# Output products of four of six token tiles in seven block products instead of eight

## The reference

```
kv  = einsum('bhsd,bhse->bhde', k, v)            # 4 batches, 8 heads, 576 positions, head size 64
out = einsum('bhsd,bhde->bhse', q, kv)
x   = out / sqrt(mean(out*out, -1) + 1e-6) * g_norm   # as 2304 tokens x 512
x   = (x @ w_a * (x @ w_b)) @ w_out              # layer 1: 512 -> 1536 -> 512
x   = (sigmoid(x @ w_gate) * (x @ w_val)) @ w_out2    # layer 2: the same sizes
```

## Time and profile before

| | |
|---|---|
| median of 3 runs | 926.57 us (923.29 to 927.03) |
| profiled execution, its own time | 924.99 us |
| its span, first to last instruction | 923.2 us |
| PE busy | 908.6 us, 98% |
| DVE busy | 542.2 us, 59% |
| ACT busy | 460.4 us, 50% |
| mean granted TensorE clock | 0.996 |

### The profile page before, as it was taken

How to read it: one execution, slowest core, us unless ns; L and a number is a source line. 1 busy time by engine, 2 the same in 40 slices (tenths; PEclk the granted TensorE clock), 3 DMA queues, 4 the chain that set the end, 5 groups by cost and what they waited for, 6 DMA issues and landing times.

```text
span 923.2 us, 14827 instructions
## 1 busy us (share of the span) xinstructions
PE 908.6 (98%) x5313; PEld 872.3 (94%) x5313; DVE 542.2 (59%) x1020; ACT 460.4 (50%) x943; POOL 17.5 (2%) x81
## 2 busy tenths in 40 slices
PE   8989999999999999999999999999999999999997
PEld 7979999999999999999999999988999988999986
DVE  1687987773555563555573778763556563555541
ACT  3677645453534453444453664563554553554531
POOL 1121000000000000000000000000000000000000
PEclk9998999999999999999999999999999999999999
DMA  9992365586534456544455464689554558453435
GB/s 236 246 238 80 120 229 211 192 291 213 206 137 178 164 184 227 198 146 154 165 174 180 160 215 161 208 305 310 180 184 138 195 175 299 178 180 139 158 129 189
DMA packets 85544, 177.13 MB, mean 192 GB/s; under 512 B 6368, under 2 KB 52448, under 8 KB 85472
## 3 DMA queue, kind: packets, MB, share of 16 engines
q1 hardware_dynamic: 85472, 176.19, 57.0%
HBM read 146.28 MB, written 29.88 MB: 191 GB/s over the span
## 4 chain that ended last, share of the span: by engine, by line
PE 91%; DVE 3%; DMA 2%; ACT 1%; issue 1%; POOL 0%; SPq 0%; POOLq 0%; DVEq 0%; ACTq 0%
PE bank L590 57%; PE bank L624 16%; PE bank L626 16%; DMA w_raw<-in_moe_w_a_dram 1%; PE bank L504 1%; DMA kv_in<-in_v_dram 1%; PE bank L520 1%; DVE sum_sq L885 1%; ACT squares L692 0%; DVE w_lo L965 0%; ACT x_hi L752 0%; PE bank L491 0%; DVE x_lo L970 0%; DVE t_raw L959 0%; ACT w_hi L738 0%
## 5 line engine op out<-in xcount | busy, mean ns | idle before, releaser
L590 PE MATMUL bank<-x_hi,w_hi 128*128 128x384 f32 x1008 | 342.6, 340 | 1.7 <-ACT kv L686 1.7
L590 PE MATMUL bank<-x_hi,w_lo 128*128 128x384 f32 x1008 | 342.4, 340 | 0.0
L590 PE MATMUL bank<-x_lo,w_hi 128*128 128x384 f32 x1008 | 341.3, 339 | 0.0
L590 PEld LDWEIGHTS bank<-x_hi,w_hi 128*128 128x128 f32 x1008 | 189.9, 188 | 7.5 <-issue 2.0
L590 PEld LDWEIGHTS bank<-x_lo,w_hi 128*128 128x128 f32 x1008 | 190.0, 188 | 6.8
L590 PEld LDWEIGHTS bank<-x_hi,w_lo 128*128 128x128 f32 x1008 | 190.0, 188 | 0.0
L624 PE MATMUL bank<-h_hi,wo 128*128 128x384 f32 x576 | 156.1, 335 | 0.4
L965 DVE TENSOR_TENSOR w_lo<-s_raw,w_hi 128x512 fp32r<-128x512 f32 x144 | 99.1, 688 | 78.9 <-ACT w_hi L738 78.7
L626 PE MATMUL bank<-wo,h_hi 128*128 128x512 f32 x432 | 139.2, 392 | 0.9 <-DVE wo L979 0.5
L965 DVE TENSOR_TENSOR w_lo<-w_raw,w_hi 128x512 fp32r<-128x512 f32 (+1 forms) x144 | 79.8, 554 | 88.9 <-ACT w_hi L738 88.8
L772 ACT ACTIVATE h_hi<-h 128x384 fp32r<-128x384 f32 x144 | 74.0, 521 | 81.3 <-PE bank L626 23.9
(11 more groups left out here) (63 smaller groups left out, 727.4 us busy)
## 6 DMA issues: line engine op xcount, KB each, us to landing
wo<-wo_dram SPq DMA_DIRECT2D x120, 512.0 KB, 5.0
s_raw<-s_dram SPq DMA_DIRECT2D x48, 512.0 KB, 4.5
s_dram<-s_raw SPq DMA_DIRECT2D x24, 512.0 KB, 5.3
wo_dram<-wo SPq DMA_DIRECT2D x24, 512.0 KB, 5.3
w_raw<-in_moe_w_a_dram SPq DMA_DIRECT2D x18, 512.0 KB, 3.5
w_raw<-in_moe_w_b_dram SPq DMA_DIRECT2D x18, 512.0 KB, 3.8
w_raw<-in_moe_w_gate_dram SPq DMA_DIRECT2D x18, 512.0 KB, 3.8
w_raw<-in_moe_w_val_dram SPq DMA_DIRECT2D x18, 512.0 KB, 3.5
```

The source lines that it names most:

```text
L590: last = pe.matmul(to[:, 0:HT], w[:, u % 2, at, c, :], xx[:, i, c, :], start=(OPENS[i] and c == 0 and n_pass == 0), stop=(c == 1 and n_pas ...
```

## The change

Tiles 1, 2, 4 and 5 ("fast" tiles) do `h @ w_out` with seven block products for eight. The tokens are cut in two halves, the features of h in two halves of six chunks (`FC`), and the 512 output columns in two halves of 256 (`DH_OUT`). `output_product(tau, i)`, i = 0 to 6, runs behind all 12 units; no unit of a fast tile has matmuls of the output product between its own. Tiles 0 and 3 keep `project`.

- A product is six steps; a fast tile has 42 steps for 24, each with its own `h_hi` and `h_lo`. In the first layer a step is two blocks of three matmuls of 384 columns, in the second three blocks of three matmuls of 256 columns.
- The four sums of h are made by VectorE in place (`sum_h`: 24 additions of 128x384 a tile), in the buffers of h and, for two of the four blocks, in x, whose tile is no longer read by then. The ring of `h_hi` and `h_lo` has 7 slots in fast tiles.
- The four sums of w_out are made once a layer in six jobs: in tile 0 or 3 behind v = 3, 5, 7 and 9, in tile 1 or 4 at v = 1 and 4. A job (`sum_wo`) is four additions of 128x256 on VectorE, in the following unit (`split_wo_sums`) one copy of 128x1024 on ScalarE and two subtractions of 128x512 on VectorE, and 256 KB x 2 of loads and a spill of 1 MB on SP's queue.
- The additions for the next tile's token sums (`sum_tokens`) move from v = 3, 5, 7, 9 to v = 8, 9, 10, 11, and one of them is made in place in x.
- c12 and c22 of a unit are added in place; the buffers `s5`, `u2` and `c_b` are gone.
- Behind the products stand, as in a unit, a seed (`out_seed`), two kept banks (`out_keep`), and two copies and two sums into the output (`out_drain` on ScalarE, `out_sum` on VectorE). The last tile's stores of the first token half wait for the seventh product.
- w_out is loaded 512 KB at a time, now one load for two steps in a fast tile: 21 loads for a fast tile instead of 24.

```diff
-    STEPS_OF_TILE = 2 * CHUNKS
+    FC = CHUNKS // 2
+    DIRECT_STEPS = 2 * CHUNKS
+    FAST_STEPS = 7 * FC
+    H_RING, H_RING_DIRECT = 7, 4
+    DH_OUT = D // 2
...
         c_a = sb("c_a", [P, 4, HT])
-        c_b = sb("c_b", [P, 2, HT])
...
+        wo = sb("wo", [P, WO_RING, 2, 2, DH_OUT], F32R)
+        h_parts = sb("h_parts", [P, H_RING, 2, HT], F32R)
+        h_hi, h_lo = h_parts[:, :, 0, :], h_parts[:, :, 1, :]
...
+        OUT_BANKS = ((6, 7), (2, 3), (4, 5))
...
+        SUMS_AT = ({3: 0, 5: 1, 7: 2, 9: 3}, {1: 4, 4: 5}, {})
...
+            def output_product(tau, i):
+
+                f, role = fast_index(tau), ROLE[i]
+                blocks = 2 if tau < TILES else 3
+                for c in range(FC):
+                    q = i * FC + c
+                    slot = wo_slot(tau, q // 2)
+                    if q % 2 == 0:
+                        pe.wait_ge(wo_loaded[slot], 16 * wo_loads(tau, q // 2))
+                    pe.wait_ge(h_lo_ready, step(tau, q) + 1)
+                    for a in range(blocks):
+                        k, to = out_part(tau, role, a)
+                        if c == 0:
+                            if i == 0:
+                                pe.wait_ge(act_drained, act_before(tau, 0))
+                                pe.wait_ge(dve_drained, dve_before(tau, 0))
+                            elif i == 1:
+
+                                pe.wait_ge(c12_ready, unit(tau, UNITS))
+                                pe.wait_ge(h21_ready, pair(tau, PAIRS))
+                            elif i == 2:
+                                pe.wait_ge(out_seed_ready, 2 * f + k + 1)
+                            elif i == 4:
+                                pe.wait_ge(out_u2_ready, 2 * f + k + 1)
+                            elif i == 5:
+                                pe.wait_ge(out_s5_ready, 2 * f + k + 1)
+                            elif i == 6:
+                                pe.wait_ge(dve_drained, dve_before(tau, 0) + k + 1)
+                        at = slice(a * P, (a + 1) * P)
+                        for n_pass, (hh, part) in enumerate(((h_hi, 0), (h_hi, 1), (h_lo, 0))):
+
+                            opens = OPENS[i] and c == 0 and n_pass == 0 and (tau < TILES or a != 1)
+                            flags = dict(start=opens, stop=(c == FC - 1 and n_pass == 2), skip_group_check=True)
+                            if tau < TILES:
+                                last = pe.matmul(to, wo[:, slot, q % 2, part, at], hh[:, h_slot(tau, q), :], **flags)
+                            else:
+                                last = pe.matmul(to, hh[:, h_slot(tau, q), at], wo[:, slot, q % 2, part, :], **flags)
+                        if c == FC - 1 and (a == blocks - 1 or a == blocks - 2):
+                            last.then_inc(acc_done, 1)
+                        elif c < FC - 1 and a == blocks - 1:
+                            last.then_inc(project_done, 1)
...
-                    behind = project(tau, v - lag) if v >= lag else iter(())
+                    behind = project(tau, v - lag) if v >= lag and not fast(tau) else iter(())
...
-                for q in range(CHUNKS - lag, STEPS_OF_TILE):
-                    for _ in project(tau, q):
-                        pass
+                if fast(tau):
+                    for i in range(7):
+                        output_product(tau, i)
+                else:
+                    for q in range(CHUNKS - lag, DIRECT_STEPS):
+                        for _ in project(tau, q):
+                            pass
...
+            def sum_h(tau, i, c):
+
+                if i == 1:
+                    dve.wait_ge(h12_ready, pair(tau, c) + 1)
+                    dve.wait_ge(h_lo_ready, step(tau, c) + 1)
+                    dve.tensor_tensor(h11_home(c), h12_home(tau, c), h11_home(c), ALU.subtract).then_inc(t1_ready, 1)
+                elif i == 3:
+                    dve.wait_ge(h22_ready, pair(tau, c) + 1)
+                    dve.wait_ge(t1_ready, fast_pair(tau, c) + 1)
+                    dve.tensor_tensor(h12_home(tau, c), h22_home(tau, c), h12_home(tau, c), ALU.subtract).then_inc(t3_ready, 1)
+                elif i == 2:
+                    dve.wait_ge(h_lo_ready, step(tau, FC + c) + 1)
+                    dve.tensor_tensor(h11_home(c), h22_home(tau, c), h11_home(c), ALU.subtract).then_inc(t2_ready, 1)
+                else:
+                    dve.wait_ge(h_lo_ready, step(tau, 2 * FC + c) + 1)
+                    dve.wait_ge(h21_ready, pair(tau, c) + 1)
+                    dve.tensor_tensor(h11_home(c), h21_home(c), h11_home(c), ALU.subtract).then_inc(t4_ready, 1)
+
             def h1_place(tau, j, f):
...
-                    if not b_unit and v and (tau or v > 2):
-                        split_h(tau, v - 1)
-                    if tau + 1 < ALL_TILES and v in (3, 5, 7, 9):
-                        sum_tokens(tau + 1, (v - 3) // 2)
+                    if v in SUMS_AT[tau % TILES]:
+                        sum_wo(tau, SUMS_AT[tau % TILES][v])
+                    if fast(tau):
+                        if not b_unit and v:
+                            split_h(tau, j - 1)
+                    else:
+                        if not b_unit and v and (tau or v > 2):
+                            split_h(tau, v - 1)
+                    if tau + 1 < ALL_TILES and v in (8, 9, 10, 11):
+                        sum_tokens(tau + 1, v - 8)
                     split_w(u + 1, 1)
                     behind(v, 3)
+                    if fast(tau) and not b_unit and v:
+                        sum_h(tau, 1, j - 1)
                     if b_unit:
...
+                    if v - 1 in SUMS_AT[tau % TILES]:
+                        split_wo_sums(tau, SUMS_AT[tau % TILES][v - 1], 0)
+                        split_wo_sums(tau, SUMS_AT[tau % TILES][v - 1], 1)
+                    if fast(tau):
+                        if not b_unit and v:
+                            sum_h(tau, 3, j - 1)
+                        continue
...
+                if fast(tau):
+                    split_h(tau, FC - 1)
+                    sum_h(tau, 1, FC - 1)
+                    sum_h(tau, 3, FC - 1)
+                    for q in range(FC, FAST_STEPS):
+                        split_h(tau, q)
+                        if q < 3 * FC:
+                            sum_h(tau, 2 if q < 2 * FC else 4, q % FC)
+                        i = q - 17
+                        if tau + 1 < ALL_TILES and i % 2 == 0 and 0 <= i // 2 < 7:
+                            split_x(tau + 1, i // 2)
+                        if q == 6 * FC:
+                            out_sum(tau, 1)
+                    out_sum(tau, 0)
+                else:
+                    split_h(tau, CHUNKS - 1)
```

More of the change, by code:

```diff
@@ L228, in acc_before @@
         def acc_before(tau, half):
-            done = 2 * tau + half
-            return sum(accs(i // (2 * TILES)) for i in range(done))
+            done = sum(14 if fast(i) else 2 * accs(i // TILES) for i in range(tau))
+            return done + half * accs(tau // TILES)
         ACT_ACCS = [[0, 2], [0, 2]]
@@ new lines, in h_raw, with out_group @@
+        def h_raw(tau, q):
+            if not fast(tau):
+                return h1[:, q % 4, :] if q < CHUNKS else h2[:, q - CHUNKS, :]
+            i, c = divmod(q, FC)
+            if i == 3:
+                return h21_home(c)
+            if i == 4:
+                return h12_home(tau, c)
+            if i == 5:
+                return h22_home(tau, c)
+            return h11_home(c)
+        def out_group(tau, role, k):
+            cols = HT if tau < TILES else (2 * DH_OUT, DH_OUT)[k]
+            return bank[OUT_BANKS[role][k]][:, 0:cols]
@@ new lines, in out_part, with out_kept, out_home @@
+        def out_part(tau, role, a):
+            if tau < TILES:
+                return a, bank[OUT_BANKS[role][a]][:, 0:HT]
+            return a // 2, bank[OUT_BANKS[role][a // 2]][:, a % 2 * DH_OUT:(a % 2 + 1) * DH_OUT]
+        def out_kept(tau, which, k):
+            at = which * TT + (k * HT if tau < TILES else k * 2 * DH_OUT)
+            cols = HT if tau < TILES else (2 * DH_OUT, DH_OUT)[k]
+            return c_a[:, :, :].rearrange("p s t -> p (s t)")[:, at:at + cols]
+        def out_home(tau, m, half, k):
+            if tau < TILES:
+                return x[:, 2 * m + k, half_tokens(tau, half)]
+            stage = out_sb if half == 0 else x[:, 0:3, half_tokens(tau, 0).start:half_tokens(tau, 0).start + D]
+            cols = slice(m * DH_OUT, (m + 1) * DH_OUT)
+            return stage[:, 0:2, cols] if k == 0 else stage[:, 2, cols]
@@ new lines, in _ @@
+                    spill_wo(tau, v - 1)
+                if fast(tau):
+                    for k in range(WO_RING, FAST_STEPS // 2):
+                        load_wo(tau, k)
+                        if k == WO_RING + 4:
+                            load_unit(unit(tau, UNITS) + 2)
+                    load_wo_raw(tau + 1, 0)
+                    store(tau, 1)
+                else:
```

(16 more changed lines are left out.)

535 lines of the change are left out of this document (377 added, 158 removed).

## The result

The changed kernel takes **902.94 us** (median of 4 runs, 901.53 to 906.77) where the kernel before takes 926.36 (4 runs, 923.29 to 927.03): a ratio of 0.976, with a 95% interval of 0.973 to 0.980, 2.4% faster. The forecast was 908, the range 897 to 922. The profiled execution took 906.77, against 907.1 in the sum, and its span is 905.1 us.

The account below looks back on a forecast made before the run. PE, busy 98%, was taken as the bound: matmul count times distance between starts. Terms -12.6, -6.7, -1.2, +1.0 and +1.6 sum to -17.9, giving 907.1 us for the profiled execution; forecast 908, range 897 to 922.

Parts of the forecast that it names:

- First layer: Output product of tiles 1 and 2: 252 matmuls of 384 columns for 288, -12.6 us for both tiles.
- Second layer: Output product of tiles 4 and 5: 378 matmuls of 256 columns for 216 of 512, -6.7 us for both.
- Rival 1: The weight load sets the pace of 256-column matmuls, 0.1755 us each; 948 us, chance 0.10.
- Rival 4: The fixed part of a matmul's time vanishes at 256 columns; 896 us, chance 0.06.
- Switch: Fast tiles lose the wait between the two token halves, 0.3 us in each of four tiles: -1.2 us.
- Seed and kept banks: Output product: the third product's wait for ScalarE's copy of the first's bank stays hidden, 5 us to spare; cost 0.
- sums of h behind the units: Output product: VectorE's splits and sums of h keep up with PE's steps, nearest to full from step 17; cost 0.
- Units: Fast tiles' units: VectorE's c22 comes late at v = 8 and 10 (0.3 us) and v = 4 (0.7): +1.0 us.
- Rival 2: c22 comes late in every fast unit, 48 units x 0.3 us; 922 us, chance 0.10.
- rival 3: VectorE is overfull in the fresh tiles, eight units losing 1 us each; 916 us, chance 0.08.
- Transfers: Fast tiles' w_out loads take 5.0 us where a slot is asked for again after 8.4; cost 0.
- The end: After the last matmul, all six last DMAs wait for both drains of the seventh product: +1.6 us.

Follow-up runs that it names:

- e8: The changed kernel with no fast tiles, so no seven products and no sums of h and w_out; 923.17 us, ratio 0.998 to the kernel before.
- e2: The kernel before with each 512-column matmul of the second layer's output product cut in two of 256; 928.37 us, ratio 1.0040 to the kernel before.
- e1: The changed kernel run again unaltered, for the spread; 903.84 us, ratio 0.978 to the kernel before.
- e9: The changed kernel once more, on one chip beside a version with three moves; 902.63 us, ratio 0.9761 to the kernel before.
- e6: The changed kernel with w_out's sixth sums job at v = 5, next units' load ahead of w_out's, first blocks' last stores awaiting their own drain; 901.67 us, ratio 0.975.

## Why the prediction was right, point by point

- **First layer, -12.6**: right, and the safest term. Sum for tile 2: -6.5, measured -7.0. Of the 7.0, 0.43 are the wait at the switch (e8), 36 x 0.1733 = 6.2 the matmuls left out. The other 0.3 is that before, 120 matmuls of the output product stood between those of units, where twelve took 9.53 - 7.42 = 2.11 us, 0.176 each, and now run at 0.1733. The term was one of count by pace, and the pace of the run was 0.1733, before as after; the 0.1755 was read from a piece that held part of the wait.
- **Second layer, -6.7**: the step that could have turned the sign. The mechanism, a line through two sizes, is right; its two points were read too high. I took 0.1755 and 0.2290 us from pieces of the chain that hold waits, and got 0.122. The distances between starts are 0.1733 and 0.2267, the line through them gives 0.1200, and that is what 256 columns take. So the count gives 216 x 0.2267 = 49.0 less 378 x 0.1200 = 45.4, -3.6 a tile. Measured by tile (tile 4: -3.7 with the stall of 0.35 in it; tile 5: -4.2 to its last matmul) it is -4.1 and -4.2; the rest are the 0.2 at the twelfth step (e8) and units at a quicker pace, twelve in 88.21 us in tile 5 where tile 2's take 89.04. The part of a matmul's time that doesn't depend on the columns is 0.013 us at each of the three sizes (0.1733 - 0.160, 0.2267 - 0.213, 0.1200 - 0.107), and not 0.015.
- **Rival 1, the weight load sets the pace** (948): fallen twice. The load still takes 192 ns by its record, and one comes every 120; e2 says it of the kernel before, +3.7 where this rival gave 79. The sentence of the Trainium skill's "TensorE: Matmul & The Clock Gate", Part 3, The mechanism, by which a load overlaps matmuls in flight only if it goes to other rows, isn't borne out here; the same section also lets a load into a background weight buffer run ahead, and no run here shows whether that is the case. The 107 ns estimated from its section LDWEIGHTS are below the 120 measured, so the runs don't speak against them, and none shows them either. **Rival 4**, no fixed part (896), has fallen too: 0.120 isn't 0.107, and e2 got longer, where it gave -9.7.
- **Switch, -1.2**: about right in sum, 2 x 0.43 and 2 x 0.2 for 4 x 0.3, but by luck. In the first layer e8 gains the 0.43 in plain tiles as well, and in the second there was no wait at the switch, but one of 0.2 at the twelfth step, which fast tiles are rid of. The paces that the two product terms rest on held part of these waits already, so they were partly counted twice.
- **Seed and kept banks; sums of h behind the units, 0**: right. 252 and 378 matmuls stand without a break.
- **Units, +1.0**: the stall at v = 4 is where it was put. VectorE in order of time, tile 4:

```profile
663.79 0.42 DVE L1360 TENSOR_TENSOR t_raw<-wo_raw 128x256 f32<-128x256 f32 x1
664.13 0.42 DVE L1360 TENSOR_TENSOR t_raw<-t_raw,wo_raw 128x256 f32<-128x256 f32 x1
664.58 0.43 DVE L1360 TENSOR_TENSOR t_raw<-wo_raw,t_raw 128x256 f32<-128x256 f32 x1
664.93 0.55 DVE L1371 TENSOR_TENSOR h_parts<-h,h_parts 128x384 fp32r<-128x384 f32 x1
665.39 0.69 DVE L1330 TENSOR_TENSOR w_lo<-s_raw,w_hi 128x512 fp32r<-128x512 f32 x1
666.00 0.55 DVE L1379 TENSOR_TENSOR h<-h 128x384 f32<-128x384 f32 x1
666.47 0.55 DVE L1493 TENSOR_TENSOR c_a<-bank,c_a 128x384 f32<-128x384 f32 x1
```

and PE, which waits for the last of them:

```profile
666.63 0.34 PE L827 MATMUL bank<-x_hi,w_lo 128*128 128x384 f32 x1
667.16 0.41 PE L827 MATMUL bank<-x_hi,w_hi 128*128 128x384 f32 x1 [0.19 <-DVE c_a L1493]
```

VectorE goes through the four sums (the rows begin with the second), the split of h, the weight split and the sum of h without idling; c22 (L1493) comes as the last. From one start to the next PE takes 0.53 us instead of 0.175: 0.35 lost, 0.35 foreseen (the unit lasts 7.71 us, in tile 1 7.75, for 7.42). The 0.3 for the token sums at v = 8 and 10 was not there.
- **Rival 2, c22 late in every fast unit** (922) and **rival 3, VectorE overfull in fresh tiles** (916): fallen. Tile 2's twelve units are one row without a wait; tile 3 takes 139.02 for 139.06.
- **Transfers, 0**: right in e1, e9 and the second layer, short by 0.9 us in the profiled execution. The step that failed is the comparison of the deadline, 8.4 us by the sum and some 8.1 by the runs, with the median landing of 5.0.
- **The end, +1.6**: the mechanism is right, the size +1.3. The six issues begin (899.39) when the two drains end (898.50 + 0.87); e6, whose first stores don't wait for both, gets 0.3 us back.
- **The whole**: from tile 1 on -17.9 was foreseen, -19.3 came in the profiled execution and -20.3 in e1, so the account was 1.4 to 2.4 us short of the gain. In the profiled execution the products with their switch and their units gave 0.7 us more than foreseen in the first layer and 1.0 in the second, the token sums and the end 0.3 each, and the transfer wait took back 0.9. That this execution's own time, 906.77, met the sum's 907.1 so closely is luck: it reached tile 1 at 225.08 us, the kernel before at 223.84, and it had the wait. The medians differ by 23.4, in the later comparisons by 20.8 and 21.9. The first two intervals (19.0 to 24.9 and 19.0 to 22.4 us) hold what the tiles show, e9's (20.7 to 23.6) lies just above its own 19.8; medians hold the start of the kernel as well, which varies by some 3 us between executions of one kernel.

## What to carry to other kernels

Where an engine is busy 98% of the time, a count of its instructions times the distance between their starts holds. Measure that distance from starts inside a run of the same form, not as a piece of the chain over its count, which can hold a wait. Where a size is new, take the line through two known ones, then check by cutting the old kernel's instructions to the new size (e2), before the algorithm is rewritten. One product less by way of sums pays only if the sums fit in what another engine has free between two deadlines: list that engine's operations up to the one that the bound waits for, as at v = 4. Set a transfer's deadline against the longest landing in the trace, not the median: here it was 8.5 us before the change.

## What the runs showed of the hardware

- Matmuls with a full load of weights for each, in a run that doesn't wait, start every 0.1200 us at 256 columns, every 0.1733 at 384 and every 0.2267 at 512, at a granted clock of 1.00: 1/2.4 ns a column and 0.013 us. The record of a load says 188 to 192 ns throughout, so it isn't the price of a load in a run.
- The units' matmuls of 384 columns are less even. The 42 of a unit take 7.42 us (0.1767 each) in every unit of tile 2, and anything from 7.28 to 7.42 in tile 5 of the changed kernel, changing from unit to unit. In e2, 96 of them behind 512 columns cut in 256 take 16.75 us, 16.96 in e8 behind 384. What sets it is open.
- Two matmuls of 256 columns for one of 512 cost 0.013 us more by these distances (0.012 over e2's whole run), and about 0.003 each pair where matmuls of another product lie between (units of 9.45 us instead of 9.42 in e2).
- Over 14.3 us with a DMA share of 0.89 (317 GB/s) a load of 512 KB took 9.0 us, the median over the kernel being 4.6.
